# Retention in sub-chunks of 64 tokens on quarters of the TensorE array, and a later z split in the last two cycles

## What is computed

```python
for t in range(S):
    state = gamma[None, :, None, None] * state + np.einsum('bhd,bhe->bhde', k[:, :, t], v[:, :, t])
    y[:, :, t] = scale * np.einsum('bhd,bhde->bhe', q[:, :, t], state)
# second: xn is x less its mean over 512 columns, divided by its deviation, times g_ln
x = x + np.maximum(xn @ w_ch1, 0.0) @ w_ch2          # 512 -> 2048 -> 512
# third: attention of 4 experts, each token adds its best two
scores = where(causal, -1e9, scale * (q @ k.T));  a = softmax(scores);  ye = a @ v @ wo[e]
out += mask[..., None] * w[:, :, kk:kk + 1] * ye
```

## Time and profile before

| | us |
|---|---|
| median of 3 runs | 453.23 (453.15 to 453.37) |
| the profiled execution | 453.5 |
| its span, first to last instruction | 451.8 |
| TensorE busy in the span | 444.0 (98%) |
| VectorE busy | 321.2 (71%) |
| GpSimd busy | 292.5 (65%) |
| ScalarE busy | 220.5 (49%) |

### The profile page before, as it was taken

How to read it: one execution, slowest core, us unless ns; L and a number is a source line. 1 busy time by engine, 2 the same in 40 slices (tenths; PEclk the granted TensorE clock), 3 DMA queues, 4 the chain that set the end, 5 groups by cost and what they waited for, 6 DMA issues and landing times.

```text
span 451.8 us, 8177 instructions
## 1 busy us (share of the span) xinstructions
PE 444.0 (98%) x2872; PEld 402.8 (89%) x2872; DVE 321.2 (71%) x669; ACT 220.5 (49%) x519; POOL 292.5 (65%) x391
## 2 busy tenths in 40 slices
PE   7999999999999999999999999999999999999997
PEld 6899998898898889889898988988999999999875
DVE  4565989668775767787776687658557878887853
ACT  3346737514532445552345145214436777777753
POOL 3766944978689499996966786641803355556650
PEclk9999999999999999999999999999999999999999
DMA  9999403222211203321121260020163543333214
GB/s 214 241 234 262 132 0 102 85 64 76 93 45 51 65 30 94 93 91 51 49 93 47 69 176 14 0 48 1 25 149 79 140 98 94 96 96 77 89 48 163
DMA packets 76520, 41.48 MB, mean 92 GB/s; under 512 B 48064, under 2 KB 70592, under 8 KB 76480
## 3 DMA queue, kind: packets, MB, share of 16 engines
q1 hardware_dynamic: 73824, 40.37, 33.2%
q10 hardware_dynamic: 2656, 0.60, 0.6%
HBM read 28.37 MB, written 3.15 MB: 70 GB/s over the span
## 4 chain that ended last, share of the span: by engine, by line
PE 91%; DVE 2%; SPq 2%; POOL 1%; DMA 1%; issue 1%; ACT 0%; POOLq 0%
PE ps L910 30%; PE ps L893 24%; PE ps L1015 8%; PE ps L1034 5%; PE ps L1068 4%; PE ps L1049 4%; PE ps L985 4%; PE ps L1092 3%; PE ps L766 2%; PE ps L753 2%; PE ps L773 2%; PE ps L743 2%; DMA raw_q<-in_q 1%; SPq L518 1%; PE ps L800 1%
## 5 line engine op out<-in xcount | busy, mean ns | idle before, releaser
L1276 ACT ACTIVATE h_t_hi<-ps 128x384 fp32r<-128x384 f32 x64 | 31.5, 492 | 128.4 <-DVE ps L1613 68.1
L910 PE MATMUL ps<-w_hi,h_t_lo 128*128 128x512 f32 x192 | 76.2, 397 | 0.0
L910 PE MATMUL ps<-w_lo,h_t_hi 128*128 128x512 f32 x192 | 75.8, 395 | 0.0
L910 PE MATMUL ps<-w_hi,h_t_hi 128*128 128x512 f32 x192 | 75.2, 392 | 0.0
L640 POOL TENSOR_TENSOR w_lo<-raw_w,w_hi 128x512 fp32r<-128x512 f32 x32 | 44.6, 1417 | 45.9 <-ACT w_hi L1224 40.5
L706 POOL TENSOR_SCALAR a<-a,inv_den,weight 128x768 f32<-128x768 f32 (+5 forms) x48 | 34.0, 718 | 52.9 <-DVE inv_den L1854 26.6
L1594 DVE SCALAR_TENSOR_TENSOR h_t_lo<-ps,h_t_hi 128x384 fp32r<-128x384 f32 x64 | 35.6, 557 | 32.6 <-ACT h_t_hi L1276 32.6
L619 POOL TENSOR_TENSOR w_lo<-w_sum,w_hi 128x256 fp32r<-128x256 f32 x60 | 44.5, 753 | 2.5
L910 PEld LDWEIGHTS ps<-w_hi,h_t_lo 128*128 128x128 f32 x192 | 36.0, 187 | 7.7
L893 PE MATMUL ps<-xq_T_lo,w_hi 128*128 128x384 f32 x120 | 40.6, 338 | 0.0
L1355 ACT ACTIVATE a<-a,neg_max 128x768 f32<-128x768 f32 (+5 forms) x48 | 32.3, 676 | 16.5 <-DVE neg_max L1835 16.5
(11 more groups left out here) (183 smaller groups left out, 1190.8 us busy)
## 6 DMA issues: line engine op xcount, KB each, us to landing
raw_w<-in_moe_w_ch SPq DMA_DIRECT2D x64, 256.0 KB, 2.8
k_twice_hi<-pj_hi SPq DMA_DIRECT2D x32, 96.0 KB, 2.2
k_twice_lo<-pj_lo SPq DMA_DIRECT2D x32, 96.0 KB, 2.2
out_y<-out_sb SPq DMA_DIRECT2D x12, 256.0 KB, 2.0
raw_k<-in_k SPq DMA_DIRECT2D x7, 384.0 KB, 5.0
raw_q<-in_q SPq DMA_DIRECT2D x7, 384.0 KB, 5.6
raw_v<-in_v SPq DMA_DIRECT2D x7, 384.0 KB, 4.1
q_both<-pj_hi SPq DMA_DIRECT2D x16, 96.0 KB, 2.1
```

The costliest lines, as they stand in the source:

```text
L910: mm = pe.matmul(acc_bank(tau), h_tile(a_, m, which)[:, u * P:(u + 1) * P], w2[b_][:, m % 2, part, :], start=(m % NG == 0 and which in ("1 ...
L1276: act.activation(h_tile("hi", m, part), part_bank(m, part), ACT.Relu).then_inc(s_hhi, 1)
```

## The change

- Retention's chunks are worked in sub-chunks of 64 tokens. scores_of makes 24 products of 64x64 outputs in place of 12 of 128x128 (the product between the second sub-chunk's queries and the first's keys is no longer there; the state carries it); chunk_outputs makes 24 with a contraction of 64, key_values 22 (for 11 sub-chunks), state_outputs 22 with a contraction of 64. Each addresses a quarter of the array: (rows of the head or sub-chunk) x (columns of the other). state_outputs uses only the two quarters on the diagonal, since the head gives both rows and columns.
- The mask is applied once an iteration, 768 elements a partition. The states are 11 steps of 64 elements, in place of 5 of 128.
- The clearing of the kv banks is gone. The mean of batch 0 goes to bank 3, that of batch 1 stays in bank 7.
- TensorE's order is scores of the first half, chunk outputs(it-1), scores of the second half, key_values, state_outputs(it-1), turn(it+1); s_y counts once an iteration, after both halves (the last iteration's halves apart). y_out copies sub-chunks instead of halves, both behind that count. The last iteration is no longer interleaved with the one before.
- The first half of first_hidden "11" runs ahead of the mean of batch 1. The scalings and hi parts of the weights move by an iteration on ScalarE, w2_hi(0) behind the first hidden parts; the four weight_lo of GpSimd go behind the last scale_pair.
- In cycles 6 and 7 the second z_split goes behind the third weighing.

```diff
+        def s_banks():
+            return ps[:, 0:2, 0:NC * SUB].rearrange("p j (c t) -> p j c t", c=NC)
+        def y_bank(it, sub, c=0):
+            if it == NIT - 1:
+                return ps[:, (2 if c < G else 0) + sub, 0:NC * SUB]
+            return ps[:, 4 + sub, 0:NC * SUB]
...
-                            sp.wait_ge(s_y, y_turn(it - RB, 1) + 1)
+                            sp.wait_ge(s_y, it - RB + 1)
...
                 scale_pair(n)
+            for name in FIRST_WEIGHTS:
+                weight_lo(0, name)
...
-                            pool.wait_ge(s_zlo, 2 * ((g - 2) // G))
+                            pool.wait_ge(s_zlo, 2 * ((g - 2) // G) - (g % G == 2 and g // G >= HALVES - 2))
...
+                if top == 0 or n // 2 + 1 >= HALVES - 2:
+                    pool.wait_ge(s_weighed, min(2 * LAST, 2 * (G * (n // 2 + 1) + 2 + top)))
...
                     z_split(2 * c - 2)
+                if 0 < c < HALVES - 2:
                     z_split(2 * c - 1)
                 weigh(G * c + 2)
+                if c >= HALVES - 2:
+                    z_split(2 * c - 1)
                 if c < HALVES - 1:
                     weigh(G * c + 3)
...
-                if n >= 1:
-                    pe.wait_ge(s_prob, 2 * n - 1 + unit // 2)
+                if n >= 1 and unit < 2:
+                    pe.wait_ge(s_prob, n)
+                if n == HP + 2 and unit == 3:
+                    pe.wait_ge(s_xc, KT)
...
+                for c in range(G * g, G * g + G):
+                    for sub in range(2):
+                        for j in range(2):
+                            mm = pe.matmul(ps[sub_rows(sub), j, chunk_cols(c)], k_t[head_rows(j), it % 2, c, sub_rows(sub)],
+                                           q_t[head_rows(j), it % 2, c, sub_rows(sub)], start=True, stop=True)
+                if g == 1:
+                    mm.then_inc(s_s, 1)
+            def chunk_outputs(it):
+                wait_loaded(pe, it, "v", 0)
+                pe.wait_ge(s_prob, it + 1)
+                if 1 <= it < NIT - 1:
+                    pe.wait_ge(s_yx, 2 * it)
+                for c in range(NC):
                     for j in range(2):
...
+                        for sub in range(2):
+                            mm = pe.matmul(y_bank(it, sub, c)[head_rows(j), chunk_cols(c)], raw["v"][sub_rows(sub), it % RB, j, c],
+                                           prob[sub_rows(sub), it % 2, j, c, :], start=(c == 0 or it == NIT - 1 and c == G),
+                                           stop=(c == 0 and sub == 0), skip_group_check=True)
+                mm.then_inc(s_within, 1)
+            STATE_ORDER = {0: ((0, 2), (1, 3), (0, 3), (1, 2), (0, 4), (1, 5), (0, 5), (1, 4), (0, 1), (1, 1)),
+                           1: ((0, 6), (1, 7), (0, 7), (1, 6), (0, 8), (1, 9), (0, 9), (1, 8), (0, 10), (1, 11), (0, 11), (1, 10))}
             def state_outputs(it, g):
...
+                if g == 0:
+                    pe.wait_ge(s_within, it + 1)
+                pe.wait_ge(s_st, states_before(it) + (2 * G - 1 if g == 0 else NS - 1))
+                for j, n in STATE_ORDER[g]:
+                    c, sub = divmod(n, 2)
+                    mm = pe.matmul(y_bank(it, sub, c)[head_rows(j), chunk_cols(c)], state[head_rows(j), it % 2, n - 1, :],
+                                   q_t[head_rows(j), it % 2, c, sub_rows(sub)], start=False, stop=True, skip_group_check=True)
+                if g == 1 or it == NIT - 1:
+                    mm.then_inc(s_y, 1)
...
             def key_values(it):
-                for g in range(2):
-                    wait_loaded(pe, it, "v", g)
+                wait_loaded(pe, it, "v", 0)
                 pe.wait_ge(s_scaled["k"], 2 * it + 2)
                 if it >= 1:
...
+                    pe.wait_ge(s_st, states_before(it))
+                for n in range(NS - 1):
+                    c, sub = divmod(n, 2)
                     for j in range(2):
-                        rows = slice(j * D, (j + 1) * D)
-                        mm = pe.matmul(kv_bank()[rows, c, rows], scaled["k"][:, it % RB, c, rows], raw["v"][:, it % RB, j, c],
+                        mm = pe.matmul(kv_bank(sub)[head_rows(j), chunk_cols(c)],
+                                       scaled["k"][sub_rows(sub), it % RB, c, head_rows(j)], raw["v"][sub_rows(sub), it % RB, j, c],
                                        start=True, stop=True)
                 mm.then_inc(s_kv, 1)
...
+            for it in range(1, NIT):
+                scores_of(it, 0)
                 if it > 1:
...
+                    chunk_outputs(it - 1)
+                scores_of(it, 1)
                 if it == HP + 1:
                     first_mean(0)
+                key_values(it)
+                for g in range(2):
+                    state_outputs(it - 1, g)
+                if it < NIT - 1:
+                    for unit in range(4):
+                        turn(it + 1, unit)
+            chunk_outputs(NIT - 1)
             for g in range(2):
...
+                state_outputs(NIT - 1, g)
...
+            first_hidden("11", "1")
+            first_mean(1)
+            first_hidden("11", "2")
+            for part in FIRST_PARTS[1:]:
                 first_hidden(part)
...
+            def y_out(it, sub):
+                act.wait_ge(s_y, it + 1)
+                act.activation(x[:, it, :, sub_rows(sub)], y_bank(it, sub).rearrange("p (c t) -> p c t", c=NC),
+                               ACT.Copy).then_inc(s_yx, 1)
+            def last_y_out(g, sub):
+                act.wait_ge(s_y, NIT + g)
+                act.activation(x[:, NIT - 1, part_of(g), sub_rows(sub)],
+                               y_bank(NIT - 1, sub, G * g)[:, G * g * SUB:G * (g + 1) * SUB].rearrange("p (c t) -> p c t", c=G),
                                ACT.Copy).then_inc(s_yx, 1)
...
-                    for g in range(2):
-                        y_out(it - 2, g)
+            for n in range(2):
                 for unit in range(4):
...
+                    turned(n, unit)
+            for it in range(1, NIT - 1):
+                for sub in range(2):
+                    y_out(it - 1, sub)
+                for unit in range(4):
+                    turned(it + 1, unit)
                 if it == HP:
                     act.wait_ge(s_gcol, 16)
+                    scale_w1(0)
+                    for name in FIRST_WEIGHTS[:2]:
+                        weight_hi(0, name)
                 if it == HP + 1:
-                    scale_w1(0)
-                    for name in FIRST_WEIGHTS:
+                    for name in FIRST_WEIGHTS[2:]:
                         weight_hi(0, name)
+                    quad_hi(0, "B11")
+                    scale_w1(1)
                 if it == HP + 2:
-                    scale_w1(1)
                     for name in ("A11", "A12", "A22"):
                         weight_hi(1, name)
...
+                    quad_hi(0, "B21")
+            for sub in range(2):
+                y_out(NIT - 2, sub)
+            for g in range(2):
+                for sub in range(2):
+                    last_y_out(g, sub)
...
+            def apply_causal(it):
+                dve.wait_ge(s_s, it + 1)
                 if it >= 2:
...
+                    dve.wait_ge(s_y, it - 1)
+                dve.tensor_tensor(prob[:, it % 2], s_banks(),
+                                  causal[:, 0:SUB].unsqueeze(1).unsqueeze(1).broadcast_to((P, 2, NC, SUB)),
                                   ALU.mult).then_inc(s_prob, 1)
             def states(it):
                 dve.wait_ge(s_kv, it + 1)
                 if it >= 2:
...
+                    dve.wait_ge(s_y, it - 1)
+                dve.tensor_copy(state[:, it % 2, 0], kv_bank(0)[:, chunk_cols(0)]).then_inc(s_st, 1)
+                for n in range(1, NS - 1):
+                    c, sub = divmod(n, 2)
+                    dve.wait_ge(s_st, states_before(it) + n)
+                    dve.tensor_tensor(state[:, it % 2, n], kv_bank(sub)[:, chunk_cols(c)], state[:, it % 2, n - 1],
                                       ALU.add).then_inc(s_st, 1)
...
-                if it == HP + 2:
+                apply_causal(it)
+                if it == HP + 1:
                     for kk in range(KT):
                         centre(0, 0, kk)
-                b, kk = divmod(it - 2, HP)
-                if 2 <= it < NIT - 1 and kk > 0:
+                states(it)
+                b, kk = divmod(it - 1, HP)
+                if kk > 0:
                     first_sum(b, kk)
...
                 if it == HP + 2:
                     quad_lo(0, "B11")
...
+            quad_lo(0, "B21")
...
-                    dve.wait_ge(s_zlo, n - 1)
+                    dve.wait_ge(s_zlo, n if n == 2 * HALVES - 2 else n - 1)
```

More of the change, by code:

```diff
@@ L174, in retention_moe_program @@
                 q_t = sb(r, "q_t", [P, 2, NC, P])
[L175 to L176 removed]
+                prob = sb(r, "prob", [P, 2, 2, NC, SUB])
+                state = sb(r, "state", [P, 2, NS - 1, D])
```

(56 more changed lines are left out.)

119 lines of the change are left out of this document (21 added, 98 removed).

## The result

The changed kernel takes 457.52 us (median of 4 runs, 456.0 to 458.21) where the kernel before takes 453.3 in the same comparison: a ratio of 1.0089 (95% interval 1.0063 to 1.0115). It is slower, by about 4 us. Its profiled execution took 456.0, with a span of 454.2; it is the fastest of the four, 1.5 us under their median. So the trace explains 456.0; the other three have no trace.

The account below looks back on a forecast made before the run. TensorE alone was taken to bound retention from 25.55 us on, the loads before 19. Sum: 453.5 - 5.2 (C earlier) + 0.75 (behind C) - 1.1 (z split) = 447.95, median 447.7; range 446.0 to 449.5, without Rival A to 452.6.

Parts of the forecast that it names:

- Will four run at once?: Whether products on four array quarters overlap fully in retention: taken as yes, 0.058 us a step (bounds 0.058 to 0.116).
- s: Time of one TensorE step, one record on each quarter or half of the array in use; taken as 0.058 us.
- Rival A: TensorE records start no faster than today's 29 ns whatever the tile; s = 0.116, time 458.6; chance 0.18.
- TensorE's work in an iteration: Scores, chunk outputs, key values and state outputs in retention together take 3.31 us, for 4.9 to 5.1 before.
- C: Start of batch 1's centring, ending retention, forecast 54.4 us; as a rival, partial overlap, s = 0.08, 451.4, chance 0.12.
- ScalarE's copies now stand in the way: Scores start 1.72 us after state outputs; TensorE idles 0.4 us each iteration, a plain one taking 5.03 us.
- VectorE: Retention's 11 state steps take 0.26 us each, 2.85 in all, first_sum 0.76; 4.7 an iteration, under 5.03.
- The loads: Loads move up by 1.8 us, v(4) out near 22.4; 0 to 1.2 us may be lost at iteration 7.
- Rival B: Four run at once but states at 0.32 a step, or the loads, hold; C near 55.9, time 449.2; chance 0.15.
- Behind C: From C to the first product, 9.37 us stays; two quad_lo beside GpSimd add 0.75 (0 to 1.5); weights are ready.
- The z split: In cycles 6 and 7 the third group's transposes no longer wait for the weighing: 1.1 us less (0.6 to 1.3).
- the 455.4: Kernel time in us if some 25 ns is the least between matmul starts, s then 0.1; no chance given.

Follow-up runs that it names:

- the kernel with one head: The changed kernel with the second head's products left out of scores, chunk outputs, key values and state outputs: 451.81 us, ratio 0.9969 to the kernel before.
- the kernel with half the loads: The changed kernel with only the first head's half of each load from iteration 3 on: 456.95 us, ratio 1.0075 to the kernel before.
- the kernel with 64 records more: The changed kernel with 64 more TensorE records in the warm-up, ahead of the first transposes: 458.91 us, ratio 1.0129 to the kernel before.
- the four kernels with one head: The kernel with one head (451.81 us); with GpSimd's first weights ahead of iteration 7 (450.41); that with loads cut (450.2); loads cut, weights behind (449.65).

## Why the prediction was wrong, point by point

- **"Will four run at once?"**: right, at s = 0.058. Chunk outputs are 0.70 us for 48 records, key values 0.64. Rival A's mechanism (29 ns a record whatever the tile) is out: these rows are 14.6 ns a multiplication. Its time, 458.6, was near the result for another reason: pages of instructions at 4.30 us are 33.6 ns for each multiplication over the whole of an iteration.
- **"TensorE's work in an iteration"** is the step that failed. It priced records by the array alone. A record also has to be fetched, and 392 records where 180 were need more pages than arrive. Of the distance from state outputs(1) to C, the forecast had 33.3 us (21.1 to 54.4), the kernel with one head 35.1, the change 42.1. So 7.0 of the 8.8 us are the supply, made longer by the loads: stops of 5.9, and 1.5 for the clock after the second, of which some is covered at the end. The page of the profile before has a part with the DMA queues, the instruction queue among them, and the prediction did not use it.
- **The clock** was not in the sum. After the stop of 2.72 us the granted clock is 0.66 over the next 5 us, so partly at the lower of its levels, 1.2 GHz. State outputs take 2.29 us there (1.25 at full clock), nine multiplications of key values 0.35 (0.13) and the transposes with the copies 2.03 (1.75): 1.5 us in all.
- **"ScalarE's copies now stand in the way"**: right in kind. From the end of state outputs (29.44) to scores (31.19) are 1.75 us, forecast 1.72. But scores then take 0.58 + 0.37 and not 0.70, their first half paced by the copies; the turn is 31.19 - 25.85 = 5.34, forecast 5.03. Four turns make 1.2 of the missing 1.8 us.
- **VectorE**: the states were right (ten additions in 2.55 us, 0.26 a step). The tail was short by 0.6: the two first_sum, forecast at 0.76 each, took 1.05 and 1.08 beside GpSimd.
- **The loads**: v(4) was issued at 24.15, not 22.4, because the first stop stands ahead of it. Rival B had the loads as what holds; with one head they cost 0.2 or 0.3 us. In the change they act by a way that no rival had, the delay of TensorE's instruction packets.
- **Behind C**: the distance stayed 9.36, and the forecast 0.75 for GpSimd's company didn't come, since GpSimd ended at C here. Where C was early, with one head, GpSimd cost 1.3 us by another way, as the wait at L925. "The first product finds these weights ready" would not have held: there the second weights ended at 64.69 and the w2 parts at 68.59, where I had 59.3 and 62.8.
- **The z split**: forecast 1.1. It measured 0.8 us alone (0.5 to 1.3), and from the first product of group(1) to the end 1.1, in the change too (454.2 - 72.50 = 381.7 against 382.8).
- **The sum**: C came 3.5 us late in place of 5.2 early, 8.7 in all; the 0.75 behind C didn't come; the median of the changed kernel lies 1.5 over its profiled execution where 0.27 under was taken. That makes the 9.8 us between 447.7 and 457.5, and the last of the three has no trace to explain it. The rivals' sums (A, C and the 455.4) also leave out, without a reason, the 0.7 us for VectorE that the forecast has.
- **The chances**: I gave the slower side 0.18, for one mechanism only, and even the wide range, which left A out, ended at 452.6. The bound of a step's time had been drawn from records on the array alone.

What stays open is why a packet goes out no sooner than about 1 us after the page before is begun even with the DMA idle, and why 1.3 us pass from its landing to its first record; and what the change would take with the DMA free of loads, which no run has.

## What to carry to other kernels

Count TensorE's instruction records for each stretch of time, not only its busy time: cutting products into tiles that run side by side shortens the array's work but multiplies the records, and below some 14 ns of array time a record with the DMA idle (3.45 to 3.73 us over 256), or 17 among loads (4.30 and 4.39), it is the fetch of the program that counts. Split an operation over quarters only where its columns are long enough to pay for its records; here 64 columns were not, and longer ones weren't run. Look at what the DMA does when a packet is asked for, not when the stop is seen. Price two independent parts of a change apart: the small reordering at the end was worth its 0.8 us, and the large one buried it.

## What the runs showed of the hardware that was not expected

- A page of 256 TensorE records (16 KB) came every 3.45 to 3.73 us with the DMA idle, and took 4.30 us in retention; quarter products on 64 columns use one up in 2.10.
- Among loads the packet of a page goes out later: 1.91 to 2.68 us after the page before was begun, against 1.12 and 1.13 with the DMA idle or nearly so, in the kernel with half the loads.
- Four quarters do run at once, in plain float32: four products' records in each 0.058 to 0.066 us. The Trainium skill ("TensorE: Matmul & The Clock Gate", "Wait — 56ns, not 53.3ns?") has some 25 ns as the least from start to start of two matmuls; here it is 2.10 us over 128, or 16 ns, on four tiles in turn, and the measurement decides.
- After a stop of 2.72 us the granted clock was 0.66 over 5 us; after the stops of 1.51 and 1.63 us it stayed at 1.00 in its stretches. In the kernel with 64 records more, the stop of 2.00 us at 56.44 was followed by 0.90 (55 to 60 us) and 0.75 (60 to 65).
- Executions differ by up to 2 us in when the first loads arrive (state outputs(1) start at 21.58, 21.88, 22.17 and 23.80 in the four kernels with one head, whose programs for TensorE are the same), so stretches were compared from that point and not from the start.
